# Host layouts turned beforehand, 500-token chunks, and a 49-row second matmul in a two-MLP kernel after agent attention

## What is computed

```python
# q, k, v: 12480 x 128; agents: 49 x 128; w_in: 128 x 2048; w_out: 2048 x 128
a2k = softmax(scale * agents @ k.T)         # over the 12480 tokens
agent_v = a2k @ v                           # 49 x 128
x = softmax(scale * q @ agents.T) @ agent_v # over the 49 agents
h = x @ w_in1
g = where(h >= 1, h, where(h <= -1, 0, (h + 1) ** 2 / 4))
y = g @ w_out1
h2 = y @ w_in2
out = (s * relu(h2) ** 2 + b) @ w_out2
```

## Time and profile before

| | |
|---|---|
| Median of 3 runs (lowest, highest) | 1188.39 us (1187.94, 1191.43) |
| Span of the profiled execution | 1189.1 us |
| PE busy | 1165.3 us, 98% |
| PEld, DVE, ACT, POOL busy | 1003.0, 954.6, 953.0, 841.0 us |
| HBM read, written | 23.39 MB, 6.39 MB |

### The profile page before, as it was taken

How to read it: one execution, slowest core, us unless ns; L and a number is a source line. 1 busy time by engine, 2 the same in 40 slices (tenths; PEclk the granted TensorE clock), 3 DMA queues, 4 the chain that set the end, 5 groups by cost and what they waited for, 6 DMA issues and landing times.

```text
span 1189.1 us, 20297 instructions
## 1 busy us (share of the span) xinstructions
PE 1165.3 (98%) x5668; PEld 1003.0 (84%) x5668; DVE 954.6 (80%) x1573; ACT 953.0 (80%) x1856; POOL 841.0 (71%) x1264
## 2 busy tenths in 40 slices
PE   9988899999999999999999999999999999999998
PEld 8986588888888888888888888888888888888886
DVE  2365888888888888888888888878888888888876
ACT  2225888888888888888888888888888888888886
POOL 2231088788778877887888788778877887887860
PEclk9999999999999999999999999999999999999999
DMA  7653000000000000000000000000000000000000
GB/s 187 193 141 95 1 1 18 1 17 18 17 0 17 17 17 0 17 17 1 17 17 17 1 17 17 17 1 17 17 0 17 17 17 0 18 9 9 1 9 17
DMA packets 12282, 30.44 MB, mean 26 GB/s; under 512 B 1529, under 2 KB 1578, under 8 KB 11962
## 3 DMA queue, kind: packets, MB, share of 16 engines
q1 hardware_dynamic: 12218, 29.78, 9.5%
HBM read 23.39 MB, written 6.39 MB: 25 GB/s over the span
## 4 chain that ended last, share of the span: by engine, by line
PE 87%; ACT 5%; issue 3%; DVE 3%; DMA 1%; ACTq 0%; SPq 0%; DVEq 0%
PE ps_h L592 7%; PE ps_h L593 7%; PE ps_h L594 7%; PE ps_o L634 7%; PE ps_y L554 7%; PE ps_o L635 7%; PE ps_o L636 7%; PE ps_y L556 7%; PE ps_h L573 7%; PE ps_y L555 7%; PE ps_h L574 7%; PE ps_h L455 2%; PE ps_h L443 2%; PE ps_job L455 2%; ACT sb_g_hi L732 1%
## 5 line engine op out<-in xcount | busy, mean ns | idle before, releaser
L1057 POOL TENSOR_TENSOR sb_g_lo<-sb_square,sb_g_hi 128x480 fp32r<-128x480 f32 x396 | 487.1, 1230 | 33.0
L917 DVE SCALAR_TENSOR_TENSOR ps_h<-sb_square,ps_h 128x480 f32<-128x480 f32 x416 | 274.6, 660 | 107.0 <-ACT sb_square L712 105.4
L732 ACT ACTIVATE sb_g_hi<-ps_h 128x480 fp32r<-128x480 f32 x416 | 238.4, 573 | 122.9 <-DVE ps_h L917 111.6
L900 DVE SCALAR_TENSOR_TENSOR sb_g_lo<-ps_h,sb_g_hi 128x480 fp32r<-128x480 f32 x416 | 273.0, 656 | 33.6 <-ACT sb_g_hi L732 24.0
L906 DVE TENSOR_SCALAR sb_below<-ps_h 128x480 f32<-128x480 f32 x400 | 262.0, 655 | 12.8 <-PE ps_h L574 10.2
L737 ACT ACTIVATE sb_relu<-ps_h 128x480 f32<-128x480 f32 x416 | 238.1, 572 | 21.4 <-PE ps_h L594 13.6
L712 ACT ACTIVATE sb_square<-sb_below 128x480 f32<-128x480 f32 x416 | 250.3, 602 | 0.9 <-DVE sb_below L906 0.4
L746 ACT ACTIVATE sb_square<-sb_relu 128x480 f32<-128x480 f32 x416 | 249.9, 601 | 0.6
L1055 POOL TENSOR_SCALAR sb_g_hi<-sb_square 128x480 fp32r<-128x480 f32 x396 | 232.4, 587 | 0.0
L1054 POOL TENSOR_TENSOR sb_gate<-sb_ones 1x1 f32<-1x1 f32 x396 | 73.8, 186 | 187.6 <-ACT sb_square L746 180.8
L554 PE MATMUL ps_y<-sb_g_hi,sb_w_out_hi 128*128 128x480 f32 x416 | 167.2, 402 | 2.4 <-DVE sb_g_lo L900 1.5
(11 more groups left out here) (114 smaller groups left out, 1484.6 us busy)
## 6 DMA issues: line engine op xcount, KB each, us to landing
sb_kv_ring<-in_k SPq DMA_DIRECT2D x13, 480.0 KB, 5.3
sb_q_ring<-in_q SPq DMA_DIRECT2D x26, 240.0 KB, 3.0
sb_kv_ring<-in_v SPq DMA_DIRECT2D x13, 480.0 KB, 5.6
out<-sb_out_ring SPq DMA_DIRECT2D x26, 240.0 KB, 2.4
sb_w_stage<-in_moe_w_in SPq DMA_DIRECT2D x1, 1024.0 KB, 7.2
sb_w_in<-in_moe_w_in SPq DMA_DIRECT2D x1, 1024.0 KB, 10.0
sb_w_stage<-in_moe_w_out SPq DMA_DIRECT2D x2, 0.5 KB, 11.6
sb_agents<-in_agents SPq DMA_DIRECT2D x1, 24.5 KB
```

Of the source, the lines that this page charges most:

```text
L732: nc.scalar.activation(g1_hi[:, place % SPLIT_RING], h1_ps[place % H1_BANKS][:, 0:W], ACT.Relu).then_inc(g1_hi_ready, 1)
L900: nc.vector.scalar_tensor_tensor(g1_lo[:, place % SPLIT_RING], h1_ps[place % H1_BANKS][:, 0:W], 0.0, as_f32(g1_hi[:, place % SPLIT_RING]), ...
L917: nc.vector.scalar_tensor_tensor(h, square1[:, place % WORK_RING], 1.0, h, ALU.min, ALU.add).then_inc(g1_summed, 1)
L1057: nc.gpsimd.tensor_tensor(g2_lo[:, place % SPLIT_RING], square, as_f32(hi), ALU.subtract).then_inc(g2_split, 1)
```

## The change

The host now gives q, k and agents turned (channels in rows, tokens in columns) and pads q to 12500 columns; v and both w_out come laid out by tiles of 128 rows, s and b as one 128 x 2 array; the output is written turned and the host turns it back. So the kernel has no transposes of K, q and the output. Chunks are 500 tokens (25 of them), in four overlapping groups of 126. K and V are 12 blocks of 1024 tokens and one of 192, with one SBUF place for each block; the products with V now have the V tile as the stationary operand and the 49 columns of exponentials as the moving one, and a product with ones per block sums the exponentials. `m_lo` has 49 rows, and the matmul with it reads rows 0 to 48 of `probs_t`.

```diff
+W = 500
+TOK = 126
+SUBS = 4
+SUB_AT = [0, TOK, 2 * TOK, W - TOK]
+KV_TILES = 8
...
-        m_lo = sb("m_lo", [ROWS, D_FF], F32R)
+        m_lo = sb("m_lo", [n_agents, D_FF], F32R)
...
-                        pe.matmul(h, m_lo[:, j * 128:(j + 1) * 128], probs_t[:, phase], start=False, stop=True).then_inc(h1_ready, 1)
+                        pe.matmul(h, m_lo[:, j * 128:(j + 1) * 128], probs_t[0:n_agents, phase], start=False, stop=True).then_inc(h1_ready, 1)
...
-                    if j == J_TURN_Q and chunk(i, phase, 1)[2]:
-                        turn_q(i + 1, (phase + 1) % IO_RING, turns + (phase + 1) // IO_RING)
...
-                        for t in range(SUBS_PER_CHUNK):
-                            mm = pe.transpose(job_ps[0:TOK, t * C:(t + 1) * C], out_t[:, t * TOK:(t + 1) * TOK], ident[:])
-                        mm.then_inc(out_turned, 1)
...
+            def score_k(n):
+                keys = k_last[:] if n == KV_BLOCKS else kv_ring[:, n]
+                rows = block_rows(n)
+                pe.wait_ge(k_loaded[n], 16)
+                at_least(pe, a_scores_kept, n - SCORE_BANKS + 1)
+                for t in range(block_tiles(n)):
+                    mm = pe.matmul(score_banks[n % SCORE_BANKS][0:rows, t * n_agents:(t + 1) * n_agents],
+                                   keys[:, t * rows:(t + 1) * rows], agents_t[:], start=True, stop=True)
+                mm.then_inc(a_scored, 1)
+
+            def sum_exp(n):
+                rows = block_rows(n)
+                pe.wait_ge(a_block_sum, n + 1)
+                pe.matmul(o_ps[:, 0:n_agents], ones[0:rows, :], a_block[0:rows, n % 2], start=(n == 0),
+                          stop=(n == KV_BLOCKS), skip_group_check=True).then_inc(a_sum_spread, 1)
+
+            def weigh_v(n):
+                rows = block_rows(n)
+                pe.wait_ge(v_loaded[n], 16)
+                pe.wait_ge(a_exp_ready, n + 1)
+                for t in range(block_tiles(n)):
+                    values = v_last_sb[:, t * C:(t + 1) * C] if n == KV_BLOCKS else kv_ring[:, n, t * C:(t + 1) * C]
+                    mm = pe.matmul(y_ps[:, 0:n_agents], values, a_scores[0:rows, n * KV_TILES + t],
+                                   start=(n == 0 and t == 0), stop=(n == KV_BLOCKS and t == LAST_TILES - 1), skip_group_check=True)
+                mm.then_inc(v_used, 1)
```

More of the change, by code:

```diff
@@ L49, with build_program @@
 IO_RING = 3
-J_TURN_Q = 1
 J_SCORES = 3
-J_TURN_OUT = 8
 J_TURN_P = 12
-CHUNKS_PER_LOAD = 2
-KV_RING = 4
+J_BIAS = 8
+W = 500
[3 more added lines that the diff above has]
+KV_TILES = 8
+LAST_TILES = 2
+LAST_TOK = 96
+SCORE_BANKS = 4
+W_PARTS = 4
 LOW = 64
-def build_program(nc, q, k, v, agents, w_in1, w_out1, w_in2, w_out2, s, b, out):
-    _, n_tokens, C = q.shape
+def build_program(nc, q, k, v, v_last, agents, w_in1, w_out1, w_in2, w_out2, s_b, out):
+    C, n_queries = q.shape
+    n_tokens = k.shape[1]
     n_agents = agents.shape[1]
@@ L313, in all_iterations, with block_rows, block_tiles, block_scores @@
                 iteration(*divmod(i, CHUNKS_PER_TRIP))
[L315 to L322, removed]
+        def block_rows(n):
+            return LAST_TOK if n == KV_BLOCKS else 128
+        def block_tiles(n):
+            return LAST_TILES if n == KV_BLOCKS else KV_TILES
+        def block_scores(n):
+            return a_scores[0:block_rows(n), n * KV_TILES:n * KV_TILES + block_tiles(n)]
+        score_banks = [h1_ps[0], h1_ps[1], h1_ps[2], h2_ps[0]]
         m_parts = [slice(0, 128), slice(128, 512)] + [slice(at, at + 512) for at in range(512, D_FF, 512)]
@@ L340, in _ @@
         def _(sp):
[L341 to L350, removed]
@@ L447, in score_k @@
-            def score_k(n, odd):
-                pe.wait_ge(k_t_even, n + 1)
-                pe.wait_ge(k_t_odd, n + 1)
-                if not isinstance(n, int) or n >= 2:
-                    pe.wait_ge(a_scores_kept, n - 1)
-                for t in range(LOAD_SUBS):
-                    mm = pe.matmul(score_banks[odd][0:TOK, t * n_agents:(t + 1) * n_agents],
-                                   k_t[:, odd, t * TOK:(t + 1) * TOK], agents_t[:], start=True, stop=True)
-                mm.then_inc(a_scored, 1)
@@ L525, in _, with keep_awake @@
-            pe.transpose(h2_ps[0][:, 0:n_agents], agent_v[:], ident[0:n_agents, 0:n_agents]).then_inc(agent_v_turned, 1)
+            def keep_awake(turns):
+                for _ in range(turns):
+                    pe.transpose(y_ps[:, 0:128], ident[:], ident[:])
+            def score_k(n):
[6 more added lines that the diff above has]
+                                   keys[:, t * rows:(t + 1) * rows], agents_t[:], start=True, stop=True)
+                mm.then_inc(a_scored, 1)
@@ new lines, in _ @@
+            pe.wait_ge(consts_ready, 2)
+            keep_awake(13)
+            pe.wait_ge(agents_loaded, 16)
+            for n in range(BLOCKS):
+                score_k(n)
+            score_q(0, 0, 0)
+            pe.wait_ge(a_max_merged, BLOCKS)
+            pe.transpose(o_ps[0:n_agents, 0:128], a_max1[:], ident[:]).then_inc(a_max_turned, 1)
+            keep_awake(6)
+            pe.wait_ge(a_max_ready, 1)
+            pe.matmul(h2_ps[1][:, 0:n_agents], a_max[:].to_broadcast([n_agents, 128]), ident[0:n_agents, 0:n_agents],
+                      start=True, stop=True).then_inc(a_max_spread, 1)
@@ L528, in _ @@
+            keep_awake(6)
+            for n in range(BLOCKS):
+                sum_exp(n)
+                if n == KV_BLOCKS:
+                    pe.wait_ge(consts_ready, 6)
+                    turn_probs(0)
+                weigh_v(n)
             pe.wait_ge(agent_v_t_ready, 2)
-            pe.wait_ge(bias_ready, 1)
             pe.wait_ge(w_in1_loaded, 16)
@@ L539, in _, with sum_w_out2 @@
                 make_m(n)
+            def sum_w_out2(j):
+                if j == J_BIAS:
+                    pe.wait_ge(w_out2_loaded, 16)
+                    pe.wait_ge(scales_loaded, 16)
+                    pe.wait_ge(m_split, 3)
+                for f in range((j - J_BIAS) * 2, (j - J_BIAS) * 2 + 2):
+                    mm = pe.matmul(o_ps[:, 0:1], w_stage[0][:, f * 128:(f + 1) * 128], s_b_cols[:, 1:2],
+                                   start=(f == 0), stop=(f == TILES - 1))
+                if j == TILES - 1:
+                    mm.then_inc(bias_summed, 1)
             def multiply_g1(i, phase, j, lag):
@@ L690, in keep_probs @@
+            for n in range(BLOCKS):
+                keep_scores(n)
+            act.wait_ge(consts_ready, 6)
+            exp_q(0)
+            for n in range(BLOCKS):
+                exp_block(n)
             def keep_probs(c, slot):
@@ L697, in _, with round_m @@
             keep_probs(0, 0)
-            for n in range(KEPT):
+            def round_m(n):
                 act.wait_ge(m_ready, n + 1)
                 nc.scalar.copy(m_hi[:, m_parts[n]], m_out(n)).then_inc(m_hi_ready, 1)
-            def keep_m(n):
-                act.wait_ge(m_ready, n + 1)
-                nc.scalar.copy(w_in1_sb[0:ROWS, m_parts[n]], m_out(n)).then_inc(m_kept, 1)
+            for n in range(KEPT):
+                round_m(n)
             def square_below(i, phase, j):
@@ new lines, in _ @@
+            for n in range(BLOCKS):
+                rows = block_rows(n)
+                dve.wait_ge(a_scores_kept, n + 1)
+                if n == 0:
+                    nc.vector.tensor_reduce(a_max1[:], by_agent(n), AX.X, ALU.max).then_inc(a_max_merged, 1)
+                else:
+                    at_least(dve, a_max_merged, n - 1)
+                    nc.vector.tensor_reduce(a_block[0:rows, n % 2], by_agent(n), AX.X, ALU.max).then_inc(a_block_max, 1)
+                    dve.wait_ge(a_block_max, n)
+                    dve.wait_ge(a_max_merged, n)
+                    nc.vector.tensor_tensor(a_max1[0:rows], a_max1[0:rows], a_block[0:rows, n % 2], ALU.max).then_inc(a_max_merged, 1)
@@ new lines, in sum_block @@
+            def sum_block(n):
+                rows = block_rows(n)
+                dve.wait_ge(a_exp_ready, n + 1)
+                at_least(dve, a_sum_spread, n - 1)
+                nc.vector.tensor_reduce(a_block[0:rows, n % 2], by_agent(n), AX.X, ALU.add).then_inc(a_block_sum, 1)
+            dve.wait_ge(a_max_spread, 1)
+            dve.wait_ge(a_max_merged, BLOCKS)
+            for n in range(BLOCKS):
+                shift_block(n)
+                if n >= 1:
+                    sum_block(n - 1)
+                if n == 1:
@@ L880, in _ @@
[L880 to L887 removed]
+            sum_block(KV_BLOCKS)
@@ L911, in iteration @@
                 for j in range(TILES):
+                    if first(i) and KEPT + j < len(m_parts):
+                        split_m(KEPT + j)
                     n, place, there = item(i, phase, j, 1)
@@ L1068, with turned, by_tile @@
     from concourse.bass_utils import run_bass_kernel_spmd
+    def turned(x, columns):
+        rows, C = x.shape
+        a = np.zeros((C, columns), dtype=x.dtype)
+        a[:, 0:rows] = x.T
```

(19 more changed lines are left out.)

451 lines of the change are left out of this document (135 added, 316 removed).

## The result

The changed kernel takes 1333.0 us (median of 4 runs, 1327.7 to 1337.8) against 1189.6 for the kernel before, run beside it: a ratio of 1.121, 95% interval 1.118 to 1.125. It is slower, as forecast (1283), but by 50 us more, and 8 us outside the range.

What follows compares the result with a forecast made beforehand. PE was taken to bound the kernel, with 87% of the span its own work. From 1189.1 us the other terms gave 1156.1, and the 49-row matmul's 126.7 made 1283; eight-in-ten range 1150 to 1325.

Steps and rivals of the forecast that it cites:

- The pause and the exposed load: At each height change around the 49-row matmul: a 0.08 us pause plus 0.085 us for an exposed weight load.
- The two halves of the forecast: All changes but the 49-row matmul, giving 1156.1 us, and the 49-row matmul in the loop, adding 126.7.
- the sum without the 49-row matmul: Whole kernel: all other terms, from K to the tail, take 1189.1 us to 1156.1.
- Rivals 1 and 2: Second matmul of h: 1, costs as before, 1156 us, chance 0.24; 2, emptied array but hidden load, 1217, chance 0.12.
- The term of the item: Loop: two height changes per item cost 0.33 us, over 384 items +126.7 us.
- Iteration 0. ACT bounds it: Iteration 0: ACT sets its time, and 500 instead of 480 columns in three operations per item add 0.9 us.
- Iteration 0 hides it behind ACT: Iteration 0: the 49-row matmul's cost stays behind ACT's work, so only 384 items pay.
- +0.9: Iteration 0: 0.9 us more for ACT's three operations per item on 500 instead of 480 columns.
- The loop without 49 rows: Iterations after 0: 41.20 us each, 24 instead of 25, together 26.5 us less.
- V at the low clock: Stage V: 222 passes at 0.205 us, 45.5 us against 28.3, so 17.2 us more.
- rival 3: Clock rises in V (or K) as well: 23 us less beside any case; chance 0.3 inside forecast's case and rival 1.

## Why the prediction was right and wrong

**Right, by its mechanism and its sign.** The pause and the exposed load on both sides of the 49-row matmul, read from one such matmul in the start, are most of what costs: 137 us of the 171 between the profiled runs with 49 and with 113 rows. The two halves of the forecast were separable, and the run with 113 rows measures the sum without the 49-row matmul: 1156.1 forecast, 1164.6 in its trace. That nearness is the sum of a start 2.4 us shorter, an iteration 0 longer by 6.9 and full iterations longer by 4.2. Rivals 1 and 2 fell; 49 rows are not free, and the load is not hidden.

**The term of the item was somewhat small.** Forecast 0.33 per item, 126.7 us; measured 0.40 in the distances of one item and 0.36 in the time, 137.4 us. The exposed load is 0.11, where I took the 0.085 by which L554's neighbour was late, and the pause 0.09 rather than 0.08.

**The step that failed is "Iteration 0. ACT bounds it", with "Iteration 0 hides it behind ACT" for the 49-row matmul.** At "+0.9" I carried over the high clock of the old iteration 0. It now runs at the low one, PE bounds it, and it takes 58.7 us instead of 31.1. I had priced the low clock in V and not asked what it does to the next stage. Of the 27.6 us, 20.7 go when 113 rows come back (58.7 to 38.0), since with them the clock rises near 114 us and ACT bounds the iteration again. The low clock also reaches into iteration 1 and costs 10 us there. Without these two terms the time would lie near 1298 us, inside the range.

What PE also does in iteration 0 costs only because PE bounds it: the eight items in which it now makes the sixteen products with w_out2 for the bias (L417), left out of the sum, are 3.5 us long in the changed kernel against 2.7 without them, some 7 us in all. With 113 rows, behind ACT, items with and without them are 1.8 to 1.9 us long.

**What the sum left out of iteration 0.** The other 6.9 us are mostly a wait that the prediction doesn't have. Before, POOL made the parts of m_lo after the first two (L1037); now DVE makes them (L690), and in its order they stand ahead of the first items' own operations. With 113 rows DVE waits 1.89, 1.01 and 2.35 us for ACT's rounding of these parts, and PE stands still 5.36 us ahead of its fourth L452, where it waited 0.53 before:

```profile
111.66 0.46 PE L573 MATMUL ps_h<-sb_probs_t,sb_m_hi 113*128 113x480 f32 x1 [0.53 <-DVE sb_g_lo L900]
...
108.77 0.76 PE L452 MATMUL ps_h<-sb_probs_t,sb_m_hi 113*128 113x500 f32 x1 [5.36 <-DVE sb_g_lo L699]
```

That matmul comes 10.9 us after the first one instead of 5.1. This is also the stretch of idle PE behind which the clock is low in all the kernels with the new start. No run gave the parts back to POOL, so what the wait costs by way of the clock stays open.

**The loop without 49 rows.** 41.2 us per iteration forecast, 993.0/24 = 41.4 measured. The 25 us by which the changed kernel's full iterations missed are so 4.2 for this, 10.7 for the term of the item and 10.1 for the low clock in iteration 1. The 500 columns stretched the distance from 0.2175 to 0.2265, where 0.2258 was taken.

**V at the low clock** was right, and rival 3 fell: 3.41 us for 16 passes is 0.213 each (0.205 taken). Here the trace also records the clock as 0.50. Before, the record said 1.00 in stage K at nearly this pace (0.1925 with 120 weight columns), so the pace of a known matmul told more than the record.

**The range** was missed because its upper end held only a longer pause (0.12), and no case in which the low clock outlives V.

## What to carry to other kernels

A matmul of 49 rows in a stream of full-height ones cost 0.36 to 0.40 us on top of its own 0.23 here, while one of 65 rows cost nothing extra. Leave such a matmul at the height of its neighbours, with rows of zeros or rows that the product can use; the fewer rows saved nothing. When a change lets PE work with few moving columns or stand still, look at the granted clock of the stage behind it too, and take the price of each matmul there at that level.

## What the runs showed of the hardware

In the changed kernel PE was recorded as busy without a break from 115 to 185 us at the low clock. Its stream held five matmuls of 500 columns per item in iteration 0 and five to eight in the first items of iteration 1, one of 49 rows among them. With the same five at 113 rows it was at the high clock within 10 us of the idle stretch. The old kernel, with 49 rows and 480 columns, was at the high clock by 115 us.

At the low clock the switch of height costs more, but not twice as much: L452, L453, L434 and L435 of iteration 0 stand 0.55, 0.72 and 0.57 apart, where 0.42 is normal at that clock (L435 to L436). That is 0.58 more for the three, against 0.40 at the high clock.

```profile
126.67 0.62 PE L452 MATMUL ps_h<-sb_probs_t,sb_m_hi 113*128 113x500 f32 x1
127.22 0.78 PE L453 MATMUL ps_h<-sb_probs_t,sb_m_lo 49*128 49x500 f32 x1
127.94 0.78 PE L434 MATMUL ps_y<-sb_g_hi,sb_w_out_hi 128*128 128x500 f32 x1
128.51 0.62 PE L435 MATMUL ps_y<-sb_g_hi,sb_w_out_lo 128*128 128x500 f32 x1
128.93 0.62 PE L436 MATMUL ps_y<-sb_g_lo,sb_w_out_hi 128*128 128x500 f32 x1
```

What decides whether the clock rises was not settled. In the kernels with the new start, 49 rows in iteration 0 decided it. But the pauses, the fewer rows and the longer distances go together there, and in the old kernel with 49 rows the clock rose in spite of all three. Its PE had stood idle for 1 us before the fall (105 to 108 us), where that of the changed kernel stood still for 3.2 us near 112.
